# Two more chunks' keys turned by VectorE and DMAs, weight loads moved behind them, three low parts a step later, another warm-up, and chunk 1's keys loaded first

## What is computed

```python
for t in range(S):
    state = alpha[:, :, t, :, None] * state + np.einsum('bhd,bhe->bhde', k[:, :, t], v[:, :, t])
    y[:, :, t] = np.einsum('bhd,bhde->bhe', q[:, :, t], state)
...
h = x @ w_in;  g = h * np.tanh(softplus(h));  x = g @ w_out      # first layer, 384 -> 2048 -> 384
h = x @ w_in;  g = h * np.cos(h);             out = g @ w_out    # second layer
```

## Time and profile before

| | |
|---|---|
| median of 3 executions | 863.65 us (863.0 to 865.07) |
| the profiled execution | 863.55 us |
| its span, first to last instruction | 861.8 us |
| TensorE busy | 854.9 us (99%) |
| VectorE busy | 428.4 us (50%) |
| ScalarE busy | 415.5 us (48%) |
| GpSimd busy | 340.8 us (40%) |
| granted TensorE clock, mean | 0.999 |

### The profile page before, as it was taken

The page is one execution under the profiler, slowest core; times in us unless marked ns, Lnnn a source line. Parts: engine busy times, 40 slices in busy tenths (PEclk is TensorE's granted clock), DMA queues, the critical chain, the costliest instruction groups (busy, mean ns, idle before and its releaser), DMA issues.

```text
span 861.8 us, 15965 instructions
## 1 busy us (share of the span) xinstructions
PE 854.9 (99%) x6316; PEld 706.2 (82%) x6316; DVE 428.4 (50%) x699; ACT 415.5 (48%) x732; POOL 340.8 (40%) x272
## 2 busy tenths in 40 slices
PE   9999999999999999999999999999999999999998
PEld 8878888888888888888888888888888888888886
DVE  8886342333414323300134666566666665665664
ACT  3644333333333333333456665565565565655654
POOL 5555344544344544322563433333333333333332
PEclk9999999999999999999999999999999999999999
DMA  8755553344444334310331200200200200200001
GB/s 301 242 156 171 148 159 96 93 135 114 129 112 139 93 101 138 100 34 32 119 94 54 75 0 1 74 1 1 74 1 0 74 1 1 73 1 1 38 0 38
DMA packets 72042, 69.25 MB, mean 80 GB/s; under 512 B 38432, under 2 KB 54048, under 8 KB 71968
## 3 DMA queue, kind: packets, MB, share of 16 engines
q1 hardware_dynamic: 71824, 68.10, 26.4%
q10 hardware_dynamic: 144, 0.13, 0.0%
HBM read 46.71 MB, written 13.63 MB: 70 GB/s over the span
## 4 chain that ended last, share of the span: by engine, by line
PE 97%; DMA 1%; DVE 1%; ACT 0%; issue 0%; SPq 0%; POOL 0%; DVEq 0%; ACTq 0%
PE low L634 45%; PE low L605 35%; PE pair L605 11%; PE pair L575 1%; PE pair L559 1%; PE low L512 1%; PE low L479 1%; DMA shared<-aqk_in 1%; PE low L493 0%; PE top L479 0%; PE top L512 0%; PE pair L460 0%; PE low L460 0%; PE low L439 0%; PE top L529 0%
## 5 line engine op out<-in xcount | busy, mean ns | idle before, releaser
L1101 POOL TENSOR_TENSOR g_lo<-g,g_hi 128x512 fp32r<-128x512 f32 x191 | 251.2, 1316 | 478.8 <-ACT g_hi L753 478.1
L605 PE MATMUL low<-x_parts,w_hi 128*128 128x512 f32 x864 | 245.2, 392 | 0.0
L634 PE MATMUL low<-g_hi,w_hi 128*128 128x512 f32 x576 | 224.6, 390 | 0.3 <-DVE x_out L988 0.3
L634 PE MATMUL low<-g_hi,w_lo 128*128 128x512 f32 x576 | 224.2, 389 | 0.0
L605 PEld LDWEIGHTS low<-x_parts,w_hi 128*128 128x128 f32 x864 | 160.5, 188 | 34.1
L753 ACT ACTIVATE g_hi<-g 128x512 fp32r<-128x512 f32 x192 | 120.7, 628 | 116.4 <-PE low L634 115.6
L634 PE MATMUL low<-g_lo,w_hi 128*128 128x512 f32 x576 | 165.8, 389 | 0.0
L634 PEld LDWEIGHTS low<-g_hi,w_hi 128*128 128x128 f32 x576 | 108.1, 188 | 23.9 <-DVE x_out L988 0.7
L634 PEld LDWEIGHTS low<-g_lo,w_hi 128*128 128x128 f32 x576 | 108.0, 188 | 22.5 <-POOL g_lo L1101 0.2
L634 PEld LDWEIGHTS low<-g_hi,w_lo 128*128 128x128 f32 x576 | 108.1, 188 | 22.4
L605 PE MATMUL low<-x_parts,w_lo 128*128 128x512 f32 x432 | 121.6, 390 | 0.0
(11 more groups left out here) (130 smaller groups left out, 800.2 us busy)
## 6 DMA issues: line engine op xcount, KB each, us to landing
w_raw<-w_in SPq DMA_DIRECT2D x32, 384.0 KB, 3.2
shared<-aqk_in SPq DMA_DIRECT2D x21, 512.0 KB, 4.1
v_sb<-v_in SPq DMA_DIRECT2D x24, 256.0 KB, 4.7
shared<-aqk_in SPq DMA_DIRECT2D x23, 258.0 KB, 4.0
mid<-x_out SPq DMA_DIRECT2D x6, 768.0 KB, 3.3
shared<-mid SPq DMA_DIRECT2D x6, 768.0 KB, 5.5
turned<-probs SPq DMA_DIRECT2D x64, 64.0 KB, 2.2
kd_t<-turned SPq DMA_DIRECT2D x16, 256.0 KB
```

The costliest lines, as they stand in the source:

```text
L605: mm = nc.tensor.matmul(bank, wp[:, f, k * P:(k + 1) * P], xp[:, j % 2, k, :], start=(n == 0), stop=(n == 3 * KT - 1))
L634: mm = nc.tensor.matmul(acc[m], wp[:, f, DM + m * P:DM + (m + 1) * P], gp[:, tile % GB, :], start=(f == 0 and n == 0), stop=(f == FT - 1 a ...
L1101: nc.gpsimd.tensor_tensor(g_lo[:, tile % GB, :], g[:, tile % GB, :], g_hi[:, tile % GB, :].bitcast(F32), ALU.subtract).then_inc(glo_ready, 1)
```

## The change

Six edits.

1. Chunks 6 and 7 join those whose keys VectorE and DMAs turn (`BY_DMA` begins at 6). `turn(6)` and `turn(7)` leave TensorE, two copies leave ScalarE, VectorE gets two block transposes (steps 6 and 9), the sync queue ten DMAs. The visits of chunks 5 and 6 take the order of the others, `inner` ahead of `scores`.
2. `lows_at`: VectorE's low parts of steps 4, 5 and 6 (pieces 7, 8, 9) are done a step later; step 4 has none, step 7 has two.
3. The sync queue issues `send_blocks` ahead of the step's weight load, no longer at the end of a step, and the weight load of step 6 moves into step 7.
4. The warm-up: `warm(10)` becomes `warm(9)`, `warm_rows(2)` becomes `warm_rows(1)`, `warm(4)` ahead of `scores(0)` becomes `spare(31)`, and `warm(1)` with `spare(17)` ahead of `scores(1)` becomes `warm(2)`.
5. `spare` goes round four tiles of 32 rows by 32 columns. This also holds for the `spare(4)` in the visit of chunk 16.
6. Chunk 1's keys and queries come in two DMAs, the keys first, as chunk 0's did.

```diff
+BY_DMA = range(BATCH + 2, CHUNKS)
...
+def lows_at(s):
+
+    visit = visit_step(BATCH + 1)
+    at = {visit - 3: [], visit - 2: [s - 1], visit - 1: [s - 1], visit: [s - 1, s]}.get(s, [s])
+    return [split_at(n) for n in at if split_at(n) is not None and lo_owner(split_at(n)) == 1]
...
-                if c == 0:
+                if c < 2:
                     sp.dma_start(qk_of(c)[:, k], aqk_in[c, :, QK_AT + QK // 2:QK_AT + QK]).then_inc(qk_in_sem[c], 16)
-                    load_a(1)
-                    sp.dma_start(qk_of(c)[:, q], aqk_in[c, :, QK_AT:QK_AT + QK // 2]).then_inc(first_q_in, 16)
+                    if c == 0:
+                        load_a(1)
+                    sp.dma_start(qk_of(c)[:, q], aqk_in[c, :, QK_AT:QK_AT + QK // 2]).then_inc(first_q_in[c], 16)
...
-                piece = split_at(s)
-                if piece is not None and piece + RAWS < 2 * FT:
-                    load_w(piece + RAWS)
+                if turned_at(s) is not None:
+                    send_blocks(turned_at(s))
+                visit = visit_step(BATCH + 1)
+                for n in {visit - 1: [], visit: [s - 1, s]}.get(s, [s]):
+                    if split_at(n) is not None and split_at(n) + RAWS < 2 * FT:
+                        load_w(split_at(n) + RAWS)
...
-                for _ in range(n):
-                    nc.tensor.matmul(bank[0:32, 480:481], ones[0:32, 0:32], ones[0:32, 0:1], start=True, stop=True)
+                for i in range(n):
+                    rows = slice(32 * (i % 4), 32 * (i % 4) + 32)
+                    nc.tensor.matmul(bank[rows, 480:481], ones[rows, 0:32], ones[rows, 0:1], start=True, stop=True)
...
-                    if next_turned(c) is not None:
-                        turn(next_turned(c))
                     halves_update(c)
                     if c == 16:
                         spare(4, banks[1])
-                    if next_turned(c) is None:
-                        inner(c)
+                    inner(c)
                     if next_scores(c) is not None:
                         scores(next_scores(c))
-                    if next_turned(c) is not None:
-                        inner(c)
                     from_states(c)
...
-            warm(10)
-            warm_rows(2)
+            warm(9)
+            warm_rows(1)
             pe.wait_ge(const_ready, 2)
             turn(0)
-            warm(4)
+            spare(31, banks[2])
             scores(0)
             turn(1)
-            warm(1)
-            spare(17, banks[2])
+            warm(2)
             scores(1)
```

37 lines of the change are left out of this document (14 added, 23 removed).

## The result

The changed kernel takes 867.22 us, the median of 16 executions (864.39 to 872.22), against 863.48 us for the kernel before in 16 executions (862.88 to 865.88). The ratio is 1.0044, with an interval of 1.0032 to 1.0056. So it is slower by 3.7 us, and above the range of the prediction.

What follows compares the result with a forecast made beforehand. TensorE was taken to bound the kernel (97% of the chain), VectorE its start. Gains of 0.70 + 0.70 + 0.38 + 0.15 = 1.93 us were to take 863.55 to 861.6 us, range 860.8 to 863.3.

Steps and rivals of the forecast that it cites:

- The visits of chunks 5 and 6: TensorE's visits without transposes: 0.70 us gained in chunk 5 (bounds 0.3 and 1.2), 0.70 in chunk 6 (0.4 and 0.75).
- VectorE's 0.5 us: Chunk 5's visit: add_first 1.31 us behind the visit's start against 0.81, so 0.5 us late, cutting 1.20 to 0.70.
- a wait or a gap besides: Chunk 5's visit in the kernel before: 0.46 us longer than chunk 6's with the same instructions, read as this.
- Chunk 16's spares: Visit of chunk 16: four spares on four tiles gain 0.15 us, bounds 0 and 0.25.
- The start: Before step 0, VectorE's list sets the pace; earlier scores from TensorE save its idle time, 0.38 us gained.
- Both idle times go: 0.38 us: Before step 0: VectorE's waits of 0.18 us ahead of chunk 0's mask and 0.20 ahead of chunk 3's vanish.
- The clock comes up late, the other side: Rival at the start: TensorE's clock stays low; 6.2 us if until 19.76, 868.2 us; chance 0.05 beyond 8.5 us, 0.06 shorter.
- The price of a spare: Start: the 62 spare records on four tiles take 0.5 to 0.9 us, between 15 and 36 ns each bounding 0.9 to 2.2.
- The start loses: Rival: spares run singly, start loses 1.0 us instead of gaining 0.38, nothing in chunk 16; 863.2 us, chance 0.12.
- Sum of these: 0: Sync queue behind the new waits: chunk 7's loads 1 us late but hidden, weight loads and chunk 6's keys covered; costs 0.

Runs made afterwards that it cites:

- e7: Changed kernel with the old warm-up, and 22 spares on four tiles for 17 on one to restore the instruction count; 865.09 us, ratio 1.0014.
- e2: Kernel before with only the new warm-up and the spares on four tiles; 867.47 us, ratio 1.004.
- e5: Kernel before with 26 spares on four tiles for 17 on one, 36 more TensorE instructions ahead of step 0; 866.67 us, ratio 1.0036.
- e9: Kernel before with warm(9) and warm_rows(1), warm(4) kept, 19 spares on four tiles for 17 on one; 863.21 us, ratio 0.9999.
- e13: Kernel before with 21 spares on four tiles for 17 on one, 16 more TensorE instructions; 863.64 us, ratio 1.0006.
- e10: Kernel before with 19 spares on four tiles for warm(4), and 2 on four tiles for the later 17, count kept; 864.42 us, ratio 1.0012.
- e6: Kernel before with the new warm-up and four-tile spares, but 22 spares for 31, so the instruction count stays as before; 864.67 us, ratio 1.0009.
- e1: Changed kernel with the old warm-up and old spares, other edits kept; 866.38 us, ratio 1.0027.
- e14: Changed kernel with warm(4) back ahead of scores(0) and 27 spares later, its instruction count kept; 866.72 us, ratio 1.0046.
- e15: Changed kernel with 27 spares for 31 ahead of scores(0), 16 TensorE instructions less; 865.75 us, ratio 1.0021.
- e8: Changed kernel with the old warm-up, 20 spares on four tiles, only chunk 6 turned by VectorE and DMAs, chunk 7 by TensorE; 861.9 us, ratio 0.9982.
- e3: Changed kernel with the old warm-up and chunk 7's keys loaded ahead of chunk 8's loads; 870.53 us, ratio 1.0076.
- e4: Changed kernel with the old warm-up, blocks and keys of chunks 6 and 7 issued by ScalarE a step later; 869.39 us, ratio 1.0063.
- e11: Changed kernel with the old warm-up, chunk 7 turned by TensorE, and chunk 16's four spares on four tiles; 861.81 us, ratio 0.998.

## Why the prediction was wrong

It forecast a gain of 1.93 us and the kernel lost 3.7. Its gains came as forecast or larger; two of its steps failed, and one mechanism was missing from it.

- **The visits of chunks 5 and 6: right, one of them undersized.** Chunk 5 gained 1.20 us, not 0.70. The step that was mis-sized is VectorE's 0.5 us: `add_first` was put 1.31 us behind the visit's start, and it came at 54.94, 0.81 behind 54.13, as in the visit that served as the measure. The two low parts took 0.93 and 1.41 us and the transposition 0.70, so VectorE gained the upper bound of 0.7 us. e7 shows the same visit at 2.29 us with an early first product, so the late start of the changed kernel isn't the reason. Chunk 6 gained 0.67 to 0.68, where 0.70 was said. Part of chunk 5's gain is not the transposes': the kernel before takes 0.46 us longer there in its profile than e2, e5, e9 and e13, which keep the transposes. The prediction called this 0.46 us "a wait or a gap besides" and counted it as gained without knowing what it was. Most of it is the gap of the instruction stream at record 1,473. It went because the change moved that record to an earlier place, which the prediction didn't foresee, and this part is luck.
- **Chunk 16's spares: right,** 0.17 us for 0.15.
- **The start: the step that failed first.** "Both idle times go: 0.38 us" held only for a clock that stays at 2.4 GHz; the first product came 2.70 us later instead. VectorE's waits for TensorE grew to 0.75 and 1.55 us. The rival that said it, "The clock comes up late, the other side", had 0.05, and its price of 6.2 us for 12.4 us of low clock was above the 2.7 us seen for 10.25 us of low clock. The prediction weighed what TensorE does *ahead* of 7 us, and e9 shows that this costs nothing. By e10 and e9 the cause lies in what replaces `warm(4)`: matmuls of one column, and then a wait. In e10 it costs 1.1 us in the median, in e6 1.4, and 0 to 2.6 in one execution. Why the same kernel keeps its clock in one execution and loses it in another stays open.
- **The price of a spare: right.** 62 records took 0.73 us, 12 ns each, where the prediction said 0.5 to 0.9, and e10's 38 took 0.48. The rival "The start loses" rested on the Trainium skill, page "TensorEngine Tiling (Array Packing)", section "Gotcha 1: PSUM Pressure". By it the spares should have run one after another, 2.2 us at the 36 ns of a single tile. They wrote one bank from four row tiles and did not.
- **"Sum of these: 0": the step that cost most.** The queue was looked at only up to the decays of chunk 7 and the keys of chunk 6, and both were covered as far as TensorE goes. Chunk 7's own keys, three steps on, were never put on it. They make two trips, one of four blocks out to DRAM and one load back, and the second begins when the first has landed. In the changed kernel the blocks landed 5.1 us behind the end of their issue, the load went out 0.7 us later and took 7.44 us; in e7 the trips took 4.8 and 9.9 us. The prediction had no time for either, and TensorE waited 2.4 us (1.9 to 2.8 in e1, e7, e14 and e15). The queue adds to it: the four block DMAs held it for 3.66 and 3.45 us in the changed kernel (2.6 to 3.7 in other versions) instead of the 2.4 assumed. The DMA engines were busy 0.62 of the time from 54 to 82 us before and 0.76 after. The return load's 4.8 us in a quiet stretch fits that the other transfers lengthen it, but no run isolates this. Shown: e8, which leaves chunk 7 to TensorE, loses nothing there, and is 3.2 us faster than e7. Two attempts at another order failed: keys first moved the delay to chunk 8's queries (e3), and ScalarE as the issuer sent everything later (e4).
- **Missing: the instruction stream.** The prediction counted instructions by what they last. e5 shows that 36 more of them at 11 us, free by themselves, cost 3.4 us in visits 130 and 220 us later, and e2 and e6 differ by 36 and 2.8 us. Those two are clear of noise. e1 and e7 differ by 20 instructions and 1.3 us, the changed kernel and e15 by 16 and 1.5 us, and 16 alone in e13 gave 0.3; these three are not. In the last four columns of the table the places of the gaps go with the count, whatever edits the kernel has: none at 0 and 2, chunk 10 at 16, chunks 10 and 15 at 36, and at -20 chunk 17 in e1, e3 and e4 and chunk 12 in e1 and e4. How long a gap is, and whether a place has one at all, differs from trace to trace. No trace shows the engine's store of instructions itself, but the list of the gaps leaves little else than that it had run out of them: always the same record but for multiples of 256, always 1.26 to 1.60 us behind a 16 KB transfer. (In chunk 5's visit e8 and e11 have the same count and differ by 0.37 us; there `from_states` of e8 waited 0.2 us for VectorE's `add_first`, and that of e11 didn't.) The Trainium skill, page "Runtime: NRT & Kernel Launch", section "Instruction fetch mechanics", describes such refills of 16 KiB blocks of 256 instructions and calls the cost of crossing one mostly hidden. Where these gaps fell it was not: 0.33 to 2.02 us each.

In medians the parts are: keys of chunk 7 3.2 us (e7 against e8), the warm-up 1.4 (e6 against before), the count 0.3 (e13) to 1.5 (e15), together 4.9 to 6.1 lost, and 1.4 gained by the version without them (e8). That makes 3.5 to 4.7 against 3.7 measured. The parts don't simply add; e15 has keys and warm-up together and loses 2.4 us, where e6 and e7 lose 1.4 and 1.8. Why e14 gained only 0.5 us in the median stays open.

## What to carry to other kernels

When work is moved to a queue that issues in order, follow it to the last user of the second and third item behind it, give every trip to DRAM and back a time of its own, and read it from the same kind of transfer under the same load. On an engine that is 99% busy with a few hundred tiny instructions at a time, the number of instructions ahead is itself a variable: before a gain or loss of a few microseconds is put down to an edit, run the kernel before with the same count. And when the filler ahead of a kernel is changed, look at the clock in many executions, since in e10 seven of twelve lost it and five did not.

## What was not expected of the hardware

- **TensorE stalled for 0.33 to 2.02 us inside visits, always at a record 193 + a multiple of 256 and 1.26 to 1.60 us behind a 16 KB transfer of the instruction queue.** 36 instructions more moved the median by 3.4 us, 16 more by 0.3.
- **The clock often fell behind or during a stop of TensorE in the middle of the kernel, but not always.** After the stall of 2.02 us in e5 it was at 1.2 GHz for 3.41 us, and behind the wait of 2.4 us in the changed kernel the mean clock was 0.56 from 85.45 to 89.30. Of the nine stops of 1.9 us and more behind step 0 in these traces, seven have such a fall. The 2.8 us in e7 and the 1.9 us in e1 have none.
- **A return load of turned keys lasts 4.8 us in a quiet stretch and up to 10.1 us with others around it;** at the 267 to 331 GB/s that the DMA engines moved at the start its 256 KB would take 0.8 to 1.0 us, an estimate.
- **Small matmuls on four tiles came at 12 ns a record though they write one bank,** against 36 ns on one tile: 62 records in 0.73 us, and 34 in 1.23.
